# Attention and MLP on one core: a second v product a pair in three passes, two low queries made on GpSimd

## The chip, the core and the metric

The kernel runs on one core of a Trainium2 chip. Its engines are PE (TensorE, matrix products into PSUM; PEld is its weight load), DVE (VectorE), ACT (ScalarE), POOL (GpSimd) and SP (SyncE, which here issues DMAs). The metric is the device time of one execution in microseconds.

## The reference

```python
q_rot, k_rot = (rotate(q), rotate(k))          # rotary embedding, halves of the 64 features
scores = scale * np.matmul(q_rot, k_rot.transpose(0, 1, 3, 2))
scores = scores - np.max(scores, axis=-1, keepdims=True)
attn = np.exp(scores)
attn = attn / (np.sum(attn, axis=-1, keepdims=True) + 1e-09)
out = np.matmul(attn, v)                       # 4 x 8 heads, 576 tokens, 64 features
...
h = x @ w_in                                   # x: 2304 tokens x 512; w_in: 512 x 1024
e = np.exp(h - np.max(h, axis=-1, keepdims=True))
solu = h * (e / (np.sum(e, axis=-1, keepdims=True) + 1e-09))
ln = (solu - mu) / np.sqrt(var + 1e-06) * g_ln
return (ln @ w_out).astype(np.float32)
```

All is fp32.

## The kernel before, in words

**Pairs and steps.** The 32 heads are taken as 16 pairs (n = 0 to 15), head a = 0 on partitions 0 to 63 and a = 1 on 64 to 127. The 576 keys of a head are four blocks of 128 and a tail of 64; the two tails share a block. That makes 9 steps a pair: s = 0 to 3 are the blocks of head 0, s = 4 (BOTH) the tails, s = 5 to 8 the blocks of head 1. In step s PE computes `score(n, s)` (L1014), ACT its exponential (`exp`, L573, the row L593), and PE, one step behind, the product of an earlier exponential with its v block (`weigh`, L1071, the row L1087). The product of step 7's exponential is k = 8 and is made in step 8. The tails' product is `weigh_tails`. Between them PE computes one block of scores of the next pair, row by query (`row_scores(n + 1, s)`, L986, row L1010), from which DVE takes maxima (`row_max`, L771, row L782). All maxima of steady pairs use one PSUM place, so a `row_scores` waits until the maximum before it is taken, on `max_taken`.

**Two numbers for one.** Queries, keys and weights are split into a rounded part and the rest, both of a type that PE takes in one pass: `high` on ACT (L536, row L541) rounds queries and keys of a pair, `second_queries` (L554, row L556) copies the rounded queries to the other head's partitions, `copy_keys` (L559) the rounded keys; `low_keys` (L751, row L757) and `low_queries` (L761, row L767) make the rest on DVE, `w_high` (L604) and `w_low` (L804, row L806) do it for the MLP's weights. The v products are unsplit fp32, two PE records for each half of the columns, but for one block a pair: `halved(n, k)` (L216) is true for k = 3 in pairs 1 to 14. There the exponential goes from one PSUM place to another (L587), ACT rounds it into p_hi (L590), DVE makes p_lo (`low_p`, L792, row L795), GpSimd has made v_hi and v_lo of that block (`halve_v`, L419), and PE runs three passes (`weigh_halves`, L1060, row L1067), after waits for all of these.

**What sets the order.** Nothing schedules at run time. Each engine runs its own list in the order of its loops, and waits on semaphores; whatever stands behind a wait waits with it. GpSimd's loop for pair n (L510) is: wait for `low_q_done[1]` of pair n + 1, multiply pair n + 2 by the rotary table (L394), divide pair n - 2's output (L434), copy the tails (`set_tails`), and `halve_v(n + 1)`. DVE's loop (L904) has, beside the maximum of each step: low_keys(n + 1, 1) in step 0, low_queries(n + 1, 1) in step 1, low_p in step 3, w_low in step 4, the rotary `add(n + 2)` in step 5, the reciprocal (`invert`) in step 6, low_keys(n + 2, 0) in step 7, low_queries(n + 2, 0) in step 8. Pair 1 has its own variants. ACT's loop (L647) has high(n + 2, 0) behind the exponential of step 6 and second_queries(n + 2, 0) behind that of step 7. SP loads the input of pair n + 3 once its buffer's reader counts are reached (`wait_x`, L258).

**After the pairs** come 18 tiles of 128 tokens through the MLP, which the change leaves alone.

Of the kernel before, what the change touches and what calls it, by code (L numbers as in the profile page):

```python
# [52 lines left out]
HALVED = 3  # L53
# [7 lines left out]
def attention_then_mlp(nc: bass.Bass, x_d, v_d, rope_d, w_d, gain_d, out_d):  # L61
# [8 lines left out]
    with ctx:  # L70
# [19 lines left out]
        v_hi = sb("v_hi", [P, P], F32R)  # L90
        v_lo = sb("v_lo", [P, P], F32R)
# [13 lines left out]
        v_hi_done = sem("v_hi_done")  # L105
        v_lo_done = sem("v_lo_done")
# [109 lines left out]
        def halved(n, k):  # L216

            return k == HALVED and 1 <= n < PAIRS - 1

# [37 lines left out]
        def _(sp):  # L257
            def wait_x(m):  # L258
                for a in range(2):
                    sp.wait_ge(hi_done[a], 2 * m - 2)  # L260
                    sp.wait_ge(low_k_done[a], m - 1)
                    sp.wait_ge(low_q_done[a], m - 1)
                if m >= 3:
                    sp.wait_ge(tails_set, 3 * (m - 2))

# [124 lines left out]
        def _(pool):  # L390
# [14 lines left out]

            def set_tails(m):
# [59 lines left out]
            nc.gpsimd.memset(v_hi[:, D:P].bitcast(F32), 1.0).then_inc(v_const, 1)  # L466
            nc.gpsimd.memset(v_lo[:, D:P].bitcast(F32), 0.0).then_inc(v_const, 1)
            pool.wait_ge(v_const, 6)
# [66 lines left out]
        def _(act):  # L535
            def high(m, a):  # L536
# [22 lines left out]
            def copy_keys(m, a):  # L559
# [3 lines left out]
                else:  # L563
                    act.wait_ge(hi_done[a], 2 * m + 1)
# [8 lines left out]
            def exp(n, s):  # L573
# [73 lines left out]
            for n in range(PAIRS):  # L647
                if 2 <= n < PAIRS - 1:
                    high(n + 1, 1)
                for s in range(STEPS):  # L650
                    exp(n, s)
                    if n == 1 and s == 0:
                        high(2, 1)
                    if n == 1 and s == 1:
                        second_queries(2, 1)
                    if n == 0:
                        if s == 2:
                            high(1, 0)
                            second_queries(1, 0)
                        if s == 3:  # L660
                            high(1, 1)
# [55 lines left out]
        def _(dve):  # L717
# [33 lines left out]
            def low_keys(m, a):  # L751
# [3 lines left out]
                else:  # L755
                    dve.wait_ge(hi_done[a], 2 * m + 1)
# [4 lines left out]
            def low_queries(m, a):  # L761
# [3 lines left out]
                if m == 2 and a == 0:  # L765
                    dve.wait_ge(low_q_done[0], 2)
# [25 lines left out]
            def low_p(n):  # L792

                dve.wait_ge(p_hi_done, n)
                nc.vector.tensor_tensor(p_lo[:, :].rearrange("p (b c) -> p b c", b=2), o_ps[1][:, :, 0:HALF],  # L795
# [97 lines left out]
            for s in range(STEPS):  # L893
# [7 lines left out]
                if s == 8:  # L901
                    low_keys(2, 0)
                    low_queries(1, 1)
            for n in range(1, PAIRS - 1):  # L904
                for s in range(STEPS):
# [17 lines left out]
                    if s == 7 and n + 2 < PAIRS:  # L923
# [49 lines left out]
        def _(pe):  # L973
# [12 lines left out]
            def row_scores(m, i):  # L986
                c, k = m % 2, STEPS * m + i
                if i == 0:
                    pe.wait_ge(hi_done[0], 2 * m + 2)
                    pe.wait_ge(low_k_done[0], m + 1)  # L990
                    pe.wait_ge(pool_const, 7)
                if i == BOTH:
                    pe.wait_ge(hi_done[1], 2 * m + 2)
# [66 lines left out]
            def weigh_halves(n):  # L1060

                pe.wait_ge(v_lo_done, n)
                pe.wait_ge(p_hi_done, n)
                pe.wait_ge(p_lo_done, n)
                for v, p in ((v_hi, p_hi), (v_lo, p_hi), (v_hi, p_lo)):
                    for half in range(2):
                        ins = nc.tensor.matmul(o_ps[0][:, half, 0:HALF], v[:, :], p[:, half * HALF:(half + 1) * HALF],  # L1067
# [3 lines left out]
            def weigh(n, k, half):  # L1071
                if halved(n, k):
                    if half == 1:
                        weigh_halves(n)
# [3 lines left out]
                if half == 0:  # L1078
                    if k == 0:
                        pe.wait_ge(v_loaded[c], uses(n) * 32)  # L1080
                        pe.wait_ge(v_const, 6)
# [136 lines left out]
```

## Time and profile before

| | before |
|---|---|
| median of 3 runs | 487.47 us (487.36 to 487.50) |
| the profiled execution's own time | 487.08 us |
| its span | 485.3 us |
| PE busy | 476.8 us (98%) |
| DVE busy | 368.7 us (76%) |
| ACT busy | 264.4 us (54%) |
| POOL busy | 191.9 us (40%) |
| PE's waits named by the profile | 4.8 us in all, none between 85 and 252 us |

The busy time of an engine is read beside the stretch it lies in: ACT's 54% is an average over the pairs, where it is near 80%, and the MLP. The page's chain of work that ended last is PE for 95% of the span. In the timelines each line gives a start, a duration, the engine, the line of the kernel, the operation with its output and inputs, and in brackets the engine's idle time before it with its releaser. PE's durations overlap, as products are pipelined, so the time that one costs is the difference of two starts.

### The profile page before, as it was taken

To read this page: it belongs to the slowest core of one execution; us is meant where nothing else is said; L and a number is where in the kernel's file an instruction comes from. 1 tells how busy PE (TensorE), PEld (TensorE's weight loads), DVE (VectorE), ACT (ScalarE), POOL (GpSimd) and SP (SyncE) were. 2 spreads that over 40 slices of the span, in tenths; PEclk is the share of its full clock that TensorE was granted. 3 is DMA by queue.
4 is the path that set the end of the run, shared out by engine and by line. 5 is a ranking of instruction groups with operands and counts; after the bars stand their busy time and mean duration, and the time that the engine had idled before them with its cause. 6 is when DMAs were issued, how large, how long until landed. Compare 5 with 4: busy or idle time off the path is not lost.

```text
span 485.3 us, 7697 instructions
## 1 busy us (share of the span) xinstructions
PE 476.8 (98%) x2527; PEld 403.1 (83%) x2527; DVE 368.7 (76%) x580; ACT 264.4 (54%) x397; POOL 191.9 (40%) x238
## 2 busy tenths in 40 slices
PE   8899999999999999999999999999999999999997
PEld 7677888988888888888888878888888888888885
DVE  6869787787778777877876356999897899888731
ACT  4667787778788778877787353033224222322221
POOL 6856356536453654565361012343343121122110
PEclk9999999999999999999999999999999999999999
DMA  8503454535454554445424112133333233322332
GB/s 291 188 12 76 138 158 110 178 123 162 117 156 143 144 148 141 155 108 166 149 72 99 39 34 52 32 65 87 81 70 86 47 54 67 80 56 60 62 77 85
DMA packets 101007, 50.58 MB, mean 104 GB/s; under 512 B 90280, under 2 KB 90280, under 8 KB 99048
## 3 DMA queue, kind: packets, MB, share of 16 engines
q1 hardware_dynamic: 100152, 50.00, 38.3%
q8 instruction: 20, 0.33, 0.3%
q10 hardware_dynamic: 816, 0.10, 0.1%
q14 instruction: 19, 0.16, 0.1%
HBM read 33.33 MB, written 4.79 MB: 79 GB/s over the span
## 4 chain that ended last, share of the span: by engine, by line
PE 95%; DVE 2%; ACT 1%; DMA 1%; POOL 1%; issue 0%; SPq 0%; DVEq 0%; POOLq 0%; ACTq 0%
PE ps L1087 22%; PE ps L1101 20%; PE ps L1115 20%; PE ps L1039 18%; PE ps L1010 8%; PE ps L1054 4%; PE ps L1067 2%; DMA X<-x_in 1%; POOL xT L394 1%; DVE nm L782 1%; DVE X L723 1%; DVE X L728 0%; ACT QK L541 0%; ACT p_main L593 0%; ACT QK L556 0%
## 5 line engine op out<-in xcount | busy, mean ns | idle before, releaser
L782 DVE TENSOR_REDUCE nm<-ps 128x1 fp32r<-128x576 f32 x144 | 108.2, 756 | 49.7 <-PE ps L1010 47.4
L1087 PE MATMUL ps<-p_main,V 128*128 128x288 f32 x456 | 129.5, 406 | 0.0
L593 ACT ACTIVATE p_main<-ps 128x576 f32<-128x576 f32 x114 | 74.2, 651 | 39.5 <-PE ps L1039 37.2
L1039 PE MATMUL ps<-QK 128*128 128x288 f32 x320 | 92.9, 371 | 0.8 <-ACT p_main L593 0.5
L394 POOL TENSOR_TENSOR X<-X,rope 128x1152 f32<-128x1152 f32 x26 | 68.7, 2665 | 59.9 <-DVE KB L767 59.7
L1101 PE MATMUL ps<-w_hi,KB 128*128 128x512 f32 x288 | 91.4, 390 | 0.0
L1115 PE MATMUL ps<-w_hi,QK 128*128 128x512 f32 x288 | 90.8, 389 | 0.0
L1087 PEld LDWEIGHTS ps<-p_main,V 128*128 128x128 f32 x456 | 80.3, 190 | 12.2 <-ACT p_main L593 0.2
L1039 PEld LDWEIGHTS ps<-QK 128*128 128x128 f32 x320 | 56.7, 189 | 19.3 <-issue 5.7
L1039 PE MATMUL ps<-KB 128*128 128x288 f32 x320 | 67.7, 293 | 0.0
L614 ACT ACTIVATE X<-ps,neg_max 128x1024 f32<-128x1024 f32 x18 | 20.1, 1119 | 83.3 <-DVE neg_max L827 83.3
L1115 PEld LDWEIGHTS ps<-w_hi,QK 128*128 128x128 f32 x288 | 54.0, 188 | 11.2
L1101 PEld LDWEIGHTS ps<-w_hi,KB 128*128 128x128 f32 x288 | 54.0, 188 | 11.1
L1010 PE MATMUL ps<-QK 128*128 128x288 f32 x260 | 57.2, 304 | 2.3 <-DVE nm L782 1.2
L448 POOL COPY V<-oe 32x256 f32<-32x256 f32 x72 | 29.7, 413 | 74.6 <-DVE QK L833 42.0
L1101 PE MATMUL ps<-w_lo,KB 128*128 128x512 f32 x144 | 56.1, 389 | 0.0
L1115 PE MATMUL ps<-w_lo,QK 128*128 128x512 f32 x144 | 56.0, 389 | 0.0
L1039 PEld LDWEIGHTS ps<-KB 128*128 128x128 f32 x320 | 51.5, 188 | 0.0
L434 POOL TENSOR_TENSOR xT<-xT,inv 128x576 f32<-128x576 f32 x16 | 23.4, 1460 | 60.0 <-DMA inv<-inv_rows 30.5
L1010 PEld LDWEIGHTS ps<-QK 128*128 128x128 f32 x260 | 40.8, 188 | 5.9 <-DVE nm L782 3.3
L438 POOL TENSOR_TENSOR r<-r,expo 128x1 f32<-128x1 f32 x18 | 16.4, 911 | 59.4 <-DVE r L856 59.4
L628 ACT ACTIVATE X<-ps 128x512 f32<-128x512 f32 x18 | 10.7, 596 | 47.7 <-PE ps L1115 42.6
(101 smaller groups left out, 646.8 us busy)
## 6 DMA issues: line engine op xcount, KB each, us to landing
X<-x_in SPq DMA_DIRECT2D x13, 1152.0 KB, 5.2
V<-oe SPq DMA_DIRECT2D x213, 32.0 KB, 1.9
V<-v_in SPq DMA_DIRECT2D x32, 160.0 KB, 2.7
out<-X SPq DMA_DIRECT2D x18, 256.0 KB, 2.3
w_raw<-w_in SPq DMA_DIRECT2D x16, 256.0 KB, 2.9
xT<-x_in SPq DMA_DIRECT2D x2, 1152.0 KB, 10.3
xT<-oe SPq DMA_DIRECT2D x16, 144.0 KB, 2.4
inv<-inv_rows SPq DMA_DIRECT2D x16, 144.0 KB, 2.9
```

Of the source, the lines that this page charges most:

```text
L394: nc.gpsimd.tensor_tensor(x, x, rope[:, :, :], ALU.mult).then_inc(done, 1)
L434: nc.gpsimd.tensor_tensor(xT[:, m, :], xT[:, m, :], inv[:, :], ALU.mult).then_inc(x_done, 1)
L448: nc.gpsimd.tensor_copy(blocks(ln_T[a], group, group), blocks(turned_l[a], group, group))\
L593: nc.scalar.activation(dst[:, :].rearrange("p (b c) -> p b c", b=2), score_ps[:, :, 0:HALF], ACT.Exp, scale=SCALE).then_inc(exp_done, 1)
L614: nc.scalar.activation(e[:, :].rearrange("p (b c) -> p b c", b=2), h_ps[t % 3], ACT.Exp, bias=neg_max[:, a:a + 1], accum_out=total[:, a:a ...
L782: nc.vector.tensor_reduce(nm[g][:, at:at + 1], src[:, :, 0:HALF], AX_XY, ALU.max, negate=True)\
L1010: ins = nc.tensor.matmul(slot[:, half, 0:HALF], queries, keys[:, half * HALF:(half + 1) * HALF], start=(g == 0), stop=(g == len(parts) - 1))
L1039: ins = nc.tensor.matmul(score_ps[:, half, 0:HALF], keys[:, of:of + P], queries[:, to + half * HALF:to + (half + 1) * HALF], start=(g == 0 ...
L1054: ins = nc.tensor.matmul(o_ps[a][:, half, 0:HALF], V[c][own(a), a, 0, :], p_tail[own(a), half * HALF:(half + 1) * HALF], start=(a == 1), s ...
L1087: ins = nc.tensor.matmul(o_ps[a][:, half, 0:HALF], v, p[:, half * HALF:(half + 1) * HALF], start=(k == 0), stop=(k == 9))
L1101: ins = nc.tensor.matmul(h_ps[t % 3][:, half, :], left[a][:, c, :], right[:, col:col + 512], start=(c == 0 and k == 0), stop=(c == KC - 1 ...
L1115: ins = nc.tensor.matmul(y_ps[a], left[a][:, c * P:(c + 1) * P], right[:, col:col + 512], start=(i == 0), stop=(i == DOWNS - 1))
```

## The change

HALVED becomes (3, 8): in pairs 1 to 14 the product k = 8 (the exponential of step 7, head 1) is made in three passes too. Its exponential goes to the other head's output place, o_ps[0]; p_hi and p_lo are shared by both products of a pair, and v_hi, v_lo exist twice. From pair 3 on, second_queries(m, 0) moves from ACT to GpSimd, with a semaphore of its own on which the first `row_scores` of a pair and the loads of x also wait. low_queries(1, 1) and low_queries(2, 0) move from DVE to GpSimd. On DVE, low_keys(n + 2, 0) goes from step 7 to step 6, pair 1's low_keys and low_queries lose their special places, and w_low(0) goes from step 4 of pair 1 to step 6, behind the reciprocal. On GpSimd the division follows the tails and the first halve_v.

```diff
-HALVED = 3
+HALVED = (3, 8)
...
+        def halves(n, a):
+
+            return 2 * (n - 1) + a + 1
+
+        def high(m, a):
+
+            return m + 4 if a == 0 and m >= 3 else 2 * m + 1
+
+        def copied(m, a):
+
+            return m + 4 if a == 0 and m >= 3 else 2 * m + 2
...
+                if m >= 5:
+                    sp.wait_ge(second_done, m - 4)
...
+            def low_queries(m, a):
+
+                c, at = m % 2, COLS[a]
+                nc.gpsimd.tensor_tensor(KB[c][own(a), 1, at:at + S], x_of(m)[own(a), 1, :],
+                                        QK[c][own(a), 0, at:at + S].bitcast(F32), ALU.subtract)\
+                  .then_inc(low_q_done[a], 1)
...
-            def halve_v(m):
+            def halve_v(m, a):
 
                 pool.wait_ge(v_loaded[m % 2], uses(m) * 32)
                 if m >= 2:
-                    pool.wait_ge(pv_done, PVS * (m - 1) + HALVED + 1)
-                    pool.wait_ge(v_lo_done, m - 1)
-                v = V[m % 2][:, 0, 1 + HALVED, 0:D]
-                nc.gpsimd.tensor_copy(v_hi[:, 0:D], v).then_inc(v_hi_done, 1)
-                pool.wait_ge(v_hi_done, m)
-                nc.gpsimd.tensor_tensor(v_lo[:, 0:D], v, v_hi[:, 0:D].bitcast(F32), ALU.subtract).then_inc(v_lo_done, 1)
-                pool.wait_ge(v_lo_done, m)
+                    pool.wait_ge(pv_done, PVS * (m - 1) + HALVED[a] + 1)
+                    pool.wait_ge(v_lo_done[a], m - 1)
+                v = V[m % 2][:, a, (HALVED[1] - 5 if a else HALVED[0] + 1), own(a)]
+                nc.gpsimd.tensor_copy(v_hi[a][:, own(a)], v).then_inc(v_hi_done[a], 1)
+                pool.wait_ge(v_hi_done[a], m)
+                nc.gpsimd.tensor_tensor(v_lo[a][:, own(a)], v, v_hi[a][:, own(a)].bitcast(F32), ALU.subtract)\
+                  .then_inc(v_lo_done[a], 1)
+                pool.wait_ge(v_lo_done[a], m)
+
+            def second_queries(m):
+
+                pool.wait_ge(score_ready, STEPS * (m - 2) + BOTH + 1)
+                nc.gpsimd.tensor_copy(QK[m % 2][other(0), 0, 0:S], x_of(m)[own(0), 1, :]).then_inc(second_done, 1)
+                pool.wait_ge(second_done, m - 2)
...
             pool.wait_ge(rot_done, 3)
-            nc.gpsimd.tensor_tensor(KB[1][own(0), 1, 0:S], x_of(1)[own(0), 1, :], QK[1][own(0), 0, 0:S].bitcast(F32),
-                                    ALU.subtract).then_inc(low_q_done[0], 1)
+            low_queries(1, 0)
+            pool.wait_ge(hi_done[1], 3)
+            pool.wait_ge(low_q_done[1], 1)
+            low_queries(1, 1)
+            pool.wait_ge(hi_done[0], 5)
+            pool.wait_ge(low_q_done[0], 2)
+            low_queries(2, 0)
             pool.wait_ge(low_q_done[0], 3)
             set_tails(2)
-            halve_v(1)
+            halve_v(1, 0)
+            halve_v(1, 1)
             for n in range(1, PAIRS):
                 if n + 2 < PAIRS:
                     pool.wait_ge(low_q_done[1], n + 2)
@@ -515,14 +551,16 @@
                     else:
                         pool.wait_ge(x_loaded[n % 2], uses(n + 2) * 16 - (16 if n % 2 else 32))
                     rotate(n + 2)
+                if n + 2 < PAIRS:
+                    pool.wait_ge(rot_done, n + 3)
+                    second_queries(n + 2)
+                    set_tails(n + 2)
+                if halved(n + 1, HALVED[0]):
+                    halve_v(n + 1, 0)
                 if n >= 2:
-                    if n + 2 < PAIRS:
-                        pool.wait_ge(rot_done, n + 3)
                     divide(n - 2)
-                if n + 2 < PAIRS:
-                    set_tails(n + 2)
-                if halved(n + 1, HALVED):
-                    halve_v(n + 1)
+                if halved(n + 1, HALVED[1]):
+                    halve_v(n + 1, 1)
...
-                if s < BOTH and halved(n, s):
-                    act.wait_ge(o_taken, 2 * n)
-                    nc.scalar.activation(o_ps[1][:, :, 0:HALF], score_ps[:, :, 0:HALF], ACT.Exp, scale=SCALE)\
+                if s != BOTH and halved(n, s + s // BOTH):
+                    a = s // BOTH
+                    act.wait_ge(o_taken, 2 * n + a)
+                    nc.scalar.activation(o_ps[1 - a][:, :, 0:HALF], score_ps[:, :, 0:HALF], ACT.Exp, scale=SCALE)\
                       .then_inc(exp_done, 1)
                     act.wait_ge(exp_done, STEPS * n + s + 1)
-                    nc.scalar.activation(p_hi[:, :].rearrange("p (b c) -> p b c", b=2), o_ps[1][:, :, 0:HALF], ACT.Copy)\
-                      .then_inc(p_hi_done, 1)
+                    nc.scalar.activation(p_hi[:, :].rearrange("p (b c) -> p b c", b=2), o_ps[1 - a][:, :, 0:HALF],
+                                         ACT.Copy).then_inc(p_hi_done, 1)
...
                     if s == (7 if n == 0 else 6) and n + 2 < PAIRS:
-                        high(n + 2, 0)
-                    if s == (8 if n == 0 else 7) and n + 2 < PAIRS:
-                        second_queries(n + 2, 0)
+                        set_high(n + 2, 0)
+                    if n == 0 and s == 8:
+                        second_queries(2, 0)
...
                     low_keys(2, 0)
-                    low_queries(1, 1)
             for n in range(1, PAIRS - 1):
                 for s in range(STEPS):
                     for place in range(3):
                         for i in maxima(n, s)[place]:
                             row_max(n + 1, i)
-                    if n == 1 and s == 0:
-                        low_queries(2, 0)
-                    if s == (1 if n == 1 else 0):
+                    if s == 0:
                         low_keys(n + 1, 1)
-                    if s == (2 if n == 1 else 1):
+                    if s == 1:
                         low_queries(n + 1, 1)
-                    if s == 4:
+                    if s == 4 and n >= 2:
                         w_low(n - 1)
-                    if s == 3 and halved(n, HALVED):
-                        low_p(n)
+                    if s == 3 and halved(n, HALVED[0]):
+                        low_p(n, 0)
+                    if s == 7 and halved(n, HALVED[1]):
+                        low_p(n, 1)
                     if s == 5 and n + 2 < PAIRS:
                         add(n + 2)
                     if s == 6:
                         invert(n - 1)
-                    if s == 7 and n + 2 < PAIRS:
+                        if n == 1:
+                            w_low(0)
+                    if s == 6 and n + 2 < PAIRS:
                         low_keys(n + 2, 0)
...
-                    pe.wait_ge(hi_done[0], 2 * m + 2)
+                    pe.wait_ge(hi_done[0], copied(m, 0))
+                    if m >= 3:
+                        pe.wait_ge(second_done, m - 2)
...
+            def weigh_halves(n, a):
+
+                pe.wait_ge(v_lo_done[a], n)
+                pe.wait_ge(p_hi_done, halves(n, a))
+                pe.wait_ge(p_lo_done, halves(n, a))
+                for v, p in ((v_hi[a], p_hi), (v_lo[a], p_hi), (v_hi[a], p_lo)):
                     for half in range(2):
-                        ins = nc.tensor.matmul(o_ps[0][:, half, 0:HALF], v[:, :], p[:, half * HALF:(half + 1) * HALF],
+                        ins = nc.tensor.matmul(o_ps[a][:, half, 0:HALF], v[:, :], p[:, half * HALF:(half + 1) * HALF],
                                                start=False, stop=False)
                 ins.then_inc(pv_done, 1)
```

DVE's list in pair 2, from the maximum of step 5 on; nm is written by a maximum, QK by low_keys, KB by low_queries, p_lo by low_p, sc by the reciprocal. Before:

```order
L782 TENSOR_REDUCE nm<-ps 128x1
L749 TENSOR_TENSOR X<-X 128x2x576
L782 TENSOR_REDUCE nm<-ps 128x1
L802 RECIPROCAL sc<-sc 128x9
L782 TENSOR_REDUCE nm<-ps 128x1
L757 TENSOR_TENSOR QK<-X,QK 64x576
L782 TENSOR_REDUCE nm<-ps 128x1
L790 STREAM_TRANSPOSE nm_row<-nm 128x32
L767 TENSOR_TENSOR KB<-X,QK 64x576
```

and of the change:

```order
L788 TENSOR_TENSOR X<-X 128x2x576
L821 TENSOR_REDUCE nm<-ps 128x1
L841 RECIPROCAL sc<-sc 128x9
L796 TENSOR_TENSOR QK<-X,QK 64x576
L821 TENSOR_REDUCE nm<-ps 128x1
L834 TENSOR_TENSOR p_lo<-ps,p_hi 128x576
L821 TENSOR_REDUCE nm<-ps 128x1
L829 STREAM_TRANSPOSE nm_row<-nm 128x32
L806 TENSOR_TENSOR KB<-X,QK 64x576
```

low_keys has passed the maximum of step 7, and low_p stands between that maximum and the one of step 8.

ACT's list in the same place, from the take-over of head 0's output (oe) on. Before:

```order
L601 ACTIVATE oe<-ps 128x576
L593 ACTIVATE p_main<-ps 128x576
L541 ACTIVATE QK<-X 64x2x576
L593 ACTIVATE p_main<-ps 128x576
L556 ACTIVATE QK<-X 64x576
L593 ACTIVATE p_main<-ps 128x576
```

and of the change:

```order
L640 ACTIVATE oe<-ps 128x576
L632 ACTIVATE p_main<-ps 128x576
L579 ACTIVATE QK<-X 64x2x576
L626 ACTIVATE ps<-ps 128x2x288
L629 ACTIVATE p_hi<-ps 128x576
L632 ACTIVATE p_main<-ps 128x576
```

The copy into p_hi stands where second_queries stood.

GpSimd's list at the start, from the second rotary product of pair 2 to that of pair 3; the numbers in the names are buffers (1 is pair 1's and pair 3's). Before:

```order
L394 TENSOR_TENSOR xT<-xT,rope 128x1152
L505 TENSOR_TENSOR KB1<-X1,QK1 64x576
L412 CAST tail_k<-xT 128x576
L414 CAST tail_q<-xT 64x64
L416 CAST tail_q<-xT 64x64
L426 CAST v_hi<-V1 128x64
L428 TENSOR_TENSOR v_lo<-V1,v_hi 128x64
```

and of the change:

```order
L409 TENSOR_TENSOR xT<-xT,rope 128x1152
L424 TENSOR_TENSOR KB1<-X1,QK1 64x576 x2
L424 TENSOR_TENSOR KB0<-xT,QK0 64x576
L434 CAST tail_k<-xT 128x576
L436 CAST tail_q<-xT 64x64
L438 CAST tail_q<-xT 64x64
L448 CAST v_hi_a<-V1 128x64
L450 TENSOR_TENSOR v_lo_a<-V1,v_hi_a 128x64
L448 CAST v_hi_b<-V1 128x64
L450 TENSOR_TENSOR v_lo_b<-V1,v_hi_b 128x64
```

Two subtractions and the second v block's pair have come in ahead of pair 3's rotary product.

## Rows read from the trace of the kernel before

**Rows 1.** One stretch with all engines' busy time; columns: engine, busy us (instructions), clock, DMA.

```profile
85.00:252.00 167.00, 167.00 (x1004) 145.67 (x1002) 130.12 (x191) 132.71 (x202) 87.98 (x82) 1.00 0.48 143
```

**Rows 2.** The timeline of PE, one pair; start us, us, engine, line, operation.

```profile
112.24 0.42 PE L1067 MATMUL ps<-p_hi,v_hi 128*128 128x288 f32 x2
...
113.03 0.43 PE L1039 MATMUL ps<-QK 128*128 128x288 f32 x2
113.30 0.42 PE L1039 MATMUL ps<-KB 128*128 128x288 f32 x2
...
118.52 0.64 PE L1039 MATMUL ps<-QK 128*128 128x288 f32 x2
119.00 0.42 PE L1039 MATMUL ps<-KB 128*128 128x288 f32 x2
119.26 0.43 PE L1010 MATMUL ps<-QK 128*128 128x288 f32 x2
119.53 1.13 PE L1087 MATMUL ps<-p_main,V 128*128 128x288 f32 x4
120.28 0.64 PE L1039 MATMUL ps<-QK 128*128 128x288 f32 x2
120.76 0.42 PE L1039 MATMUL ps<-KB 128*128 128x288 f32 x2
```

**Rows 3.** The timeline of ACT, the same pair.

```profile
109.86 0.64 ACT L587 ACTIVATE ps<-ps 128x576 f32<-128x576 f32 x1 [0.41 <-PE ps L1039]
110.53 0.65 ACT L590 ACTIVATE p_hi<-ps 128x576 fp32r<-128x576 f32 x1
...
116.47 1.15 ACT L541 ACTIVATE QK<-X 64x1152 fp32r<-64x1152 f32 x1
117.69 0.65 ACT L593 ACTIVATE p_main<-ps 128x576 f32<-128x576 f32 x1
118.36 0.69 ACT L556 ACTIVATE QK<-X 64x576 fp32r<-64x576 f32 x1
```

**Rows 4.** The timeline of DVE, the same pair.

```profile
111.21 0.76 DVE L795 TENSOR_TENSOR p_lo<-ps,p_hi 128x576 fp32r<-128x576 f32 x1 [0.32 <-ACT p_hi L590]
...
113.46 0.75 DVE L806 SCALAR_TENSOR_TENSOR w_lo<-w_raw,gain,w_hi 128x512 fp32r<-128x512 f32 x1
...
116.87 0.20 DVE L802 RECIPROCAL sc<-sc 128x9 f32<-128x9 f32 x1
117.96 0.76 DVE L782 TENSOR_REDUCE nm<-ps 128x1 fp32r<-128x576 f32 x1 [0.89 <-PE ps L1010]
118.75 0.75 DVE L757 TENSOR_TENSOR QK<-X,QK 64x576 fp32r<-64x576 f32 x1
```

**Rows 5.** The timeline of DVE, one other pair, the slowest of this row.

```profile
168.73 0.98 DVE L757 TENSOR_TENSOR QK<-X,QK 64x576 fp32r<-64x576 f32 x1
```

**Rows 6.** The timeline of POOL there.

```profile
168.44 0.66 POOL L412 CAST tail_k<-X 128x576 fp32r<-128x576 f32 x1
```

**Rows 7.** The timeline of PE at the start of pair 1 and in it.

```profile
36.87 0.50 PE L1010 MATMUL ps<-QK 128*128 128x288 f32 x2
...
48.83 0.54 PE L1010 MATMUL ps<-QK 128*128 128x288 f32 x2 [0.89 <-DVE nm L782]
49.20 1.13 PE L1087 MATMUL ps<-p_main,V 128*128 128x288 f32 x4
```

**Rows 8.** The timeline of DVE there.

```profile
36.02 0.75 DVE L757 TENSOR_TENSOR QK<-xT,QK 64x576 fp32r<-64x576 f32 x1
...
45.51 2.60 DVE L806 SCALAR_TENSOR_TENSOR w_lo<-w_raw,gain,w_hi 128x512 fp32r<-128x512 f32 x1
```

**Rows 9.** The timeline of POOL at the start.

```profile
32.34 1.41 POOL L505 TENSOR_TENSOR KB<-X,QK 64x576 fp32r<-64x576 f32 x1 [2.56 <-DVE xT L743]
...
44.92 2.64 POOL L394 TENSOR_TENSOR xT<-xT,rope 128x1152 f32<-128x1152 f32 x1
```

**Rows 10.** The page's costliest groups: GpSimd's products with the rotary table, and its waits.

```profile
L394 POOL TENSOR_TENSOR X<-X,rope 128x1152 f32<-128x1152 f32 x26 | 68.7, 2665 | 59.9 <-DVE KB L767 59.7
```

More of the change, by code:

```diff
@@ L89, in attention_then_mlp @@
         p_lo = sb("p_lo", [P, S], F32R)
-        v_hi = sb("v_hi", [P, P], F32R)
-        v_lo = sb("v_lo", [P, P], F32R)
+        v_hi = [sb(f"v_hi_{h}", [P, P], F32R) for h in "ab"]
+        v_lo = [sb(f"v_lo_{h}", [P, P], F32R) for h in "ab"]
         oe = [sb(f"oe{c}", [P, 2, S]) for c in range(2)]
@@ L104, in attention_then_mlp @@
         p_lo_done = sem("p_lo_done")
-        v_hi_done = sem("v_hi_done")
-        v_lo_done = sem("v_lo_done")
+        v_hi_done = [sem(f"v_hi_{h}_done") for h in "ab"]
+        v_lo_done = [sem(f"v_lo_{h}_done") for h in "ab"]
+        second_done = sem("second_done")
         x_loaded = [sem(f"x_loaded{c}") for c in range(2)]
@@ L216, in halved @@
         def halved(n, k):
-            return k == HALVED and 1 <= n < PAIRS - 1
+            return k in HALVED and 1 <= n < PAIRS - 1
+        def halves(n, a):
[4 more added lines that the diff above has]
+            return m + 4 if a == 0 and m >= 3 else 2 * m + 2
         def last_pair(t):
@@ L259, in wait_x @@
                 for a in range(2):
-                    sp.wait_ge(hi_done[a], 2 * m - 2)
+                    sp.wait_ge(hi_done[a], copied(m - 2, a))
                     sp.wait_ge(low_k_done[a], m - 1)
@@ L465, in _ @@
                 nc.gpsimd.memset(V[c][:, 1, :, 0:D], 1.0).then_inc(v_const, 1)
-            nc.gpsimd.memset(v_hi[:, D:P].bitcast(F32), 1.0).then_inc(v_const, 1)
-            nc.gpsimd.memset(v_lo[:, D:P].bitcast(F32), 0.0).then_inc(v_const, 1)
-            pool.wait_ge(v_const, 6)
+            for a in range(2):
+                nc.gpsimd.memset(v_hi[a][:, other(a)].bitcast(F32), 1.0).then_inc(v_const, 1)
+                nc.gpsimd.memset(v_lo[a][:, other(a)].bitcast(F32), 0.0).then_inc(v_const, 1)
+            pool.wait_ge(v_const, 8)
             nc.gpsimd.memset(expo[:, :], -0.5).then_inc(const_done, 1)
@@ L535, in _, with set_high @@
         def _(act):
-            def high(m, a):
+            def set_high(m, a):
                 c, at = m % 2, COLS[a]
@@ L563, in copy_keys @@
                 else:
-                    act.wait_ge(hi_done[a], 2 * m + 1)
+                    act.wait_ge(hi_done[a], high(m, a))
                 nc.scalar.activation(KB[c][own(a), 0, at:at + S], QK[c][own(a), 1, at:at + S].bitcast(F32), ACT.Copy)\
@@ L648, in _ @@
                 if 2 <= n < PAIRS - 1:
-                    high(n + 1, 1)
+                    set_high(n + 1, 1)
                 for s in range(STEPS):
@@ L652, in _ @@
                     if n == 1 and s == 0:
-                        high(2, 1)
+                        set_high(2, 1)
                     if n == 1 and s == 1:
@@ L657, in _ @@
                         if s == 2:
-                            high(1, 0)
+                            set_high(1, 0)
                             second_queries(1, 0)
                         if s == 3:
-                            high(1, 1)
+                            set_high(1, 1)
                         if s == 4:
@@ L755, in low_keys @@
                 else:
-                    dve.wait_ge(hi_done[a], 2 * m + 1)
+                    dve.wait_ge(hi_done[a], high(m, a))
                 nc.vector.tensor_tensor(QK[c][other(a), 1, at:at + S], x_of(m)[own(a), 3, :],
@@ L764, in low_queries @@
                     dve.wait_ge(hi_done[a], 2)
-                if m == 2 and a == 0:
-                    dve.wait_ge(low_q_done[0], 2)
+                if m == 2 + (1 - a):
+                    dve.wait_ge(low_q_done[a], m)
                 nc.vector.tensor_tensor(KB[c][own(a), 1, at:at + S], x_of(m)[own(a), 1, :],
@@ L790, in row_max, with low_p @@
                     nc.vector.transpose(nm_row[g][:, :], nm[g][:, :].bitcast(F32)).then_inc(turned[g], 1)
-            def low_p(n):
-                dve.wait_ge(p_hi_done, n)
-                nc.vector.tensor_tensor(p_lo[:, :].rearrange("p (b c) -> p b c", b=2), o_ps[1][:, :, 0:HALF],
+            def low_p(n, a):
+                dve.wait_ge(p_hi_done, halves(n, a))
+                nc.vector.tensor_tensor(p_lo[:, :].rearrange("p (b c) -> p b c", b=2), o_ps[1 - a][:, :, 0:HALF],
                                         p_hi[:, :].bitcast(F32).rearrange("p (b c) -> p b c", b=2), ALU.subtract)\
@@ L992, in row_scores @@
                 if i == BOTH:
-                    pe.wait_ge(hi_done[1], 2 * m + 2)
+                    pe.wait_ge(hi_done[1], copied(m, 1))
                     pe.wait_ge(low_k_done[1], m + 1)
@@ L1058, in weigh_tails @@
                             ins.then_inc(pv_done, 1)
[L1060 to L1065, printed above, removed]
+            def weigh_halves(n, a):
[3 more added lines that the diff above has]
+                for v, p in ((v_hi[a], p_hi), (v_lo[a], p_hi), (v_hi[a], p_lo)):
                     for half in range(2):
-                        ins = nc.tensor.matmul(o_ps[0][:, half, 0:HALF], v[:, :], p[:, half * HALF:(half + 1) * HALF],
+                        ins = nc.tensor.matmul(o_ps[a][:, half, 0:HALF], v[:, :], p[:, half * HALF:(half + 1) * HALF],
                                                start=False, stop=False)
@@ L1073, in weigh @@
                     if half == 1:
-                        weigh_halves(n)
+                        weigh_halves(n, k // 5)
                     return
@@ L1080, in weigh @@
                         pe.wait_ge(v_loaded[c], uses(n) * 32)
-                        pe.wait_ge(v_const, 6)
+                        pe.wait_ge(v_const, 8)
                         pe.wait_ge(max_taken, STEPS)
```

## The prediction, made before the result was known

> **What bounds the kernel now.** I read the table of busy time by stretches first. From 85 to 252 us PE is busy 167.00 of 167.00 us at the full granted clock, while DVE has 130, ACT 133 and POOL 88 [rows 1]. So in the attention part every microsecond of a pair is PE's; the other engines count only where PE would have to stand for them. The timeline of PE gives the price of each piece, the difference between one start and the next. The timelines of ACT and DVE in the same pair give the chain that makes the three-pass product's operands. Last come the start of pair 1, where PE does stand [rows 7], and what GpSimd waits for [rows 10].
>
> **The saving of a second product in halves.** An ordinary v product takes 119.53 to 120.28 = 0.75, and the score row behind it 0.48 (120.28 to 120.76) [rows 2]. The product in three passes takes 112.24 to 113.03 = 0.79, and the row behind it only 0.27 (113.03 to 113.30). So 1.23 becomes 1.06: 0.17 saved in each of 14 pairs (1 to 14), 2.4 us if nothing waits. Between 0 and 2.4 the rows leave no other reading, as both forms stand in the same pair.
>
> **What it needs, and when.** The product for block 8 is due at 119.53, right behind score(n,8) (118.52) and the key-row product of the next pair (119.26) [rows 2]. Its exponential is that of step 7, which starts at 117.69 [rows 3], as soon as score(n,7) is there. In the existing case the exponential starts at 109.86, its rounded copy at 110.53, the difference on DVE at 111.21, ending 111.97 [rows 3, 4]: 2.11 us from start to end. Step 4 gives that case cover, because score(n,4) has two sets of passes and the halves come at 112.24. Step 8 has one set: 117.69 + 2.11 = 119.80, and PE is ready at 119.53. So the cover is too short by 0.27 even with a free DVE.
>
> DVE is not free. The order of before has maximum(7), then low_keys(n+2,0), at 117.96 and 118.75 [rows 4]. The change puts low_keys in step 6, ahead of maximum(7). It must wait for ACT's rounding of that pair, 116.47 + 1.15 = 117.62 [rows 3], long after the reciprocal ends at 117.07 [rows 4]. So low_keys runs 117.65 to 118.40, maximum(7) 118.43 to 119.19 instead of 117.96 to 118.72, low_p 119.22 to 119.98. (ACT's copy ends 118.36 + 0.65 = 119.01, earlier.) Both maxima and low_p are queued behind the waiting low_keys, and PE waits for both: the key-row product at 119.26 needs maximum(7), taken by 119.25, just in time; the halves need low_p, 0.06 after its end (0.03 to 0.1: ACT to DVE is 0.03 in [rows 3, 4], DVE's end at 36.77 to PE's start at 36.87 is 0.1 in [rows 7, 8]): 120.04. After a wait PE's first pair of passes takes 0.37, not 0.26 (48.83 to 49.20 [rows 7]; 0.26 from 119.00 to 119.26 without one [rows 2]). So three passes 0.90, the next score row's first 0.27: 121.21 against 120.76. **Each of pairs 2 to 13 loses 0.45 net, 12 x 0.45 = 5.4 us.** Bounds for one pair: +0.17 (no wait of DVE and no slower restart: 119.86 + 0.79 + 0.27 = 120.92) and +0.68 (low_keys at 0.98, its slowest row [rows 5], instead of 0.75). I take the middle, since 0.75 is the usual duration. Pair 14 has no low_keys: 119.86 + 0.90 + 0.27 = 121.03, +0.27.
>
> **ACT, at nothing.** Its second_queries (0.69 at 118.36 [rows 3]) goes from exactly the place where the copy of 0.65 comes. exp(8) at 119.46 is not touched.
>
> **GpSimd in the steady pairs, at nothing.** It gets second_queries (64x576, one input), a second rounding and difference of a v block, and the division comes after the first rounding. It stands idle 59.7 us in 12 waits for low_queries ahead of its rotary products [rows 10], about 5 a pair. The three new operations are not in the trace; each is no larger than its subtraction of 64x576 with two inputs, 1.41 [rows 9], so together at most 4.2, which fits (and at least nothing); I take them as covered. second_queries(n+2) is needed only by the first key-row product of the next pair. Were this cover gone, the next add would come late and with it ACT's rounding. The x loads' added wait in SP is for the same rounding a pair earlier. The two extra small fills at the start lie in GpSimd's idle time.
>
> **The start.** The weights' difference w_low(0) stands at 45.51 and takes 2.60 [rows 8], beside GpSimd's product that runs to 47.56 [rows 9]; in a steady pair it takes 0.75, at 113.46 [rows 4]. PE therefore idles 0.89 at 48.83, and restarts 0.10 slower [rows 7]. Moving it behind the reciprocal takes this away: -0.99. But two subtractions of 1.41 each [rows 9] now follow the one at 32.34 on GpSimd: 33.8 to 35.2 and 35.3 to 36.7. DVE's low_keys(2,0), at 36.02 [rows 8], falls into the second. By the w_low row, which ended 0.55 after GpSimd's, it ends at 37.25 instead of 36.77; PE's product at 36.87 [rows 7] is waiting for it: +0.5 (bounds 0 and 0.7). Start together -0.5.
>
> In words of the Trainium skill, GPSIMD Engine Reference, section 1 (Specifications): the engine shares its SBUF interfaces with VectorE and contends with VectorE instructions that have two SBUF inputs. The 2.60 us row agrees. By that rule the queries made on GpSimd are not a free relief for DVE but hold up low_keys(2,0); without it the start would be worth -0.99 and not -0.5.
>
> Pair 1 in its step 6 has w_low(0) of 0.75 between the reciprocal and low_keys. It fills the 0.55 in which DVE would wait for ACT (117.07 to 117.62) and runs 0.2 over: 0.45 + 0.2 = +0.65.
>
> **Sum.** 5.4 + 0.27 + 0.65 - 0.5 = +5.8 on the profiled execution's own 487.08 (span 485.3 and 1.78 around it): 492.9. The median of the runs is 0.39 above it, which would make 493.3; I say 493.0. In the second part of the program PE goes on without waits, so the shift arrives whole.
>
> **Rivals.**
> - *DVE in time*: low_keys gets done before it matters, and only the short cover of step 8 is left. For it: pair 14 is so. Against: ACT's rounding ends at 117.62 by its row. 14 x 0.27 = 3.8, less 0.5: 490.4. Chance 0.17.
> - *Contention in the loop*: low_keys now meets GpSimd's casts each time and takes 0.98. For it: the slow row [rows 5] begins beside such a cast [rows 6]. Against: 0.75 in most pairs beside the same work. 13 pairs at 0.68, pair 14 0.27, pair 1 0.2 more, less 0.5: +8.8, 495.9. Chance 0.13.
> - *Faster*: the halves of block 8 find their operands ready. It decides in favour once low_p ends by 119.47, 0.5 before what I work out; then 14 x 0.17 and 0.5 are saved: 484.2. For it: the first halves never wait in the trace. Against: they have a step of twice the scores ahead of them. Chance 0.09.
> - *Nothing comes of it*, gains and waits cancel: 487. Chance 0.03.
> - *Larger*: GpSimd becomes late with second_queries or with the v halves, and the first key-row product waits as well, 1 us a pair: above 498. Chance 0.04.
> - My forecast, 0.54; its own range is 491.6 to 494.4 (0.1 a pair either way).
>
> A change of under 0.2% (1 us) can't be told from none here. Faster has 0.09, within 0.2% 0.04, slower 0.87. The range 489.5 to 497 takes in the first two rivals and leaves out some 0.16.
>
> **What would show it.** PE waiting some 0.5 us ahead of the halves of block 8 with low_p as the releaser, in 14 pairs; a DVE order of low_keys, maximum(7), low_p without idle time; a pair's time on PE up by 0.45 us; no wait of 0.89 in pair 1 but a later first key-row product of pair 2. PE without those waits and pairs 0.17 us shorter would prove me wrong.

## The result, and the profile after

The changed kernel takes 492.24 us (median of 6 runs, 492.05 to 492.57), the kernel before 487.48 (6 runs beside it): ratio 1.0097, 95% interval 1.0086 to 1.0107. It is slower by 4.8 us. The profiled execution has a span of 490.2 us against 485.3.

From the page of the changed kernel, the busy time and the chain that ended last:

```profile
PE 477.9 (97%) x2555; PEld 403.7 (82%) x2555; DVE 376.8 (77%) x592; ACT 263.9 (54%) x398; POOL 218.9 (45%) x283
...
PE 84%; DVE 8%; ACT 4%; issue 2%; DMA 1%; SPq 0%; ACTq 0%; DVEq 0%
```

PE's busy time has hardly moved (477.9 against 476.8, and overlapping durations blur it), but the chain, 95% PE before, now runs for 8% through DVE and for 4% through ACT. PE's waits in the changed kernel (engine, line, waited for; us in total, times, longest):

```profile
PE ps L1109 <- DVE p_lo L834: 3.2, 14, 0.3
PE ps L1052 <- ACT QK L589: 1.5, 1, 1.5
...
PE ps L1052 <- DVE nm L821: 0.6, 2, 0.3
...
PE ps L1052 <- issue: 0.5, 1, 0.5
```

There is one new wait in 14 pairs: the three-pass product (L1109) for p_lo. Where before none stood between 85 and 252 us [rows 1], each pair has one, of 0.22 us in the steady pairs. The timeline of PE, steps 4 and 8 of a steady pair of the changed kernel:

```profile
113.47 0.42 PE L1109 MATMUL ps<-p_hi,v_hi_a 128*128 128x288 f32 x2
113.73 0.43 PE L1109 MATMUL ps<-p_hi,v_lo_a 128*128 128x288 f32 x2
114.00 0.42 PE L1109 MATMUL ps<-p_lo,v_hi_a 128*128 128x288 f32 x2
114.27 0.43 PE L1081 MATMUL ps<-QK 128*128 128x288 f32 x2
114.54 0.42 PE L1081 MATMUL ps<-KB 128*128 128x288 f32 x2
...
119.75 0.64 PE L1081 MATMUL ps<-QK 128*128 128x288 f32 x2
120.23 0.42 PE L1081 MATMUL ps<-KB 128*128 128x288 f32 x2
120.49 0.53 PE L1052 MATMUL ps<-QK 128*128 128x288 f32 x2
121.25 0.50 PE L1109 MATMUL ps<-p_hi,v_hi_b 128*128 128x288 f32 x2 [0.22 <-DVE p_lo L834]
121.58 0.42 PE L1109 MATMUL ps<-p_hi,v_lo_b 128*128 128x288 f32 x2
121.84 0.43 PE L1109 MATMUL ps<-p_lo,v_hi_b 128*128 128x288 f32 x2
122.11 0.42 PE L1081 MATMUL ps<-QK 128*128 128x288 f32 x2
122.37 0.42 PE L1081 MATMUL ps<-KB 128*128 128x288 f32 x2
```

The product of block 3 at 113.47 is as [rows 2] has it: 0.80 to the next score row, which takes 0.27. The one of block 8 ought to follow the key-row product at 120.49 by 0.27 and comes 0.76 behind it, so 0.49 late, of which the record names 0.22 as idle. From score(n,8) to the second part of the next score row, 119.75 to 122.37, is 2.62 us, where [rows 2] has 118.52 to 120.76 = 2.24. ACT and DVE in the same pair:

```profile
117.71 1.15 ACT L579 ACTIVATE QK<-X 64x1152 fp32r<-64x1152 f32 x1
118.92 0.64 ACT L626 ACTIVATE ps<-ps 128x576 f32<-128x576 f32 x1
119.59 0.65 ACT L629 ACTIVATE p_hi<-ps 128x576 fp32r<-128x576 f32 x1
```

```profile
117.43 0.76 DVE L821 TENSOR_REDUCE nm<-ps 128x1 fp32r<-128x576 f32 x1
118.11 0.21 DVE L841 RECIPROCAL sc<-sc 128x9 f32<-128x9 f32 x1
118.89 0.75 DVE L796 TENSOR_TENSOR QK<-X,QK 64x576 fp32r<-64x576 f32 x1 [0.58 <-ACT QK L579]
119.68 0.76 DVE L821 TENSOR_REDUCE nm<-ps 128x1 fp32r<-128x576 f32 x1
120.35 0.75 DVE L834 TENSOR_TENSOR p_lo<-ps,p_hi 128x576 fp32r<-128x576 f32 x1
121.06 0.76 DVE L821 TENSOR_REDUCE nm<-ps 128x1 fp32r<-128x576 f32 x1
```

On DVE low_keys (L796) waits 0.58 us for ACT's rounding, and behind it stand the maximum and low_p without a gap; low_p ends at 121.10 and PE starts at 121.25. This answers to [rows 3, 4], where DVE was idle 0.89 us ahead of the maximum. Counted from one product of block 3 to the next, a pair takes 17.03 us (17.00 to 17.04 in 12 intervals) instead of 16.66.

### The profile page after: what moved, and what is told of

Its sections match the earlier page's. It is cut to its first block, busy times and chain, and to the rows that moved or that the text cites. A ratio compares the mean times of both kernels' runs of the same rounds, so it can differ in the third digit from the quotient of the medians.

```text
span 490.2 us, 7879 instructions
## 1 busy us (share of the span) xinstructions
PE 477.9 (97%) x2555; PEld 403.7 (82%) x2555; DVE 376.8 (77%) x592; ACT 263.9 (54%) x398; POOL 218.9 (45%) x283
## 4 chain that ended last, share of the span: by engine, by line
PE 84%; DVE 8%; ACT 4%; issue 2%; DMA 1%; SPq 0%; ACTq 0%; DVEq 0%
PE ps L1143 20%; PE ps L1157 20%; PE ps L1081 15%; PE ps L1129 14%; PE ps L1052 6%; PE ps L1109 5%; PE ps L1096 4%; ACT QK L579 3%; DVE nm L821 3%; DVE QK L796 2%; DVE p_lo L834 2%; DMA X<-x_in 1%; DVE X L762 1%; ACT p_main L632 0%; DVE X L767 0%
## 5 line engine op out<-in xcount | busy, mean ns | idle before, releaser
L1129 PE MATMUL ps<-p_main,V 128*128 128x288 f32 x400 | 113.6, 406 | 0.0
L1081 PE MATMUL ps<-QK 128*128 128x288 f32 x320 | 89.8, 362 | 0.8 <-ACT p_main L632 0.5
L632 ACT ACTIVATE p_main<-ps 128x576 f32<-128x576 f32 x100 | 65.0, 650 | 43.5 <-PE ps L1081 42.2
L1129 PEld LDWEIGHTS ps<-p_main,V 128*128 128x128 f32 x400 | 70.4, 190 | 10.7 <-ACT p_main L632 0.2
L1081 PEld LDWEIGHTS ps<-QK 128*128 128x128 f32 x320 | 55.9, 189 | 17.8 <-issue 5.7
L1052 PE MATMUL ps<-QK 128*128 128x288 f32 x260 | 58.2, 308 | 2.9 <-ACT QK L589 1.5
L1052 PEld LDWEIGHTS ps<-QK 128*128 128x128 f32 x260 | 40.6, 188 | 7.1 <-DVE nm L821 2.5
L866 DVE TENSOR_REDUCE neg_max<-ps 128x1 f32<-128x1024 f32 x18 | 21.6, 1199 | 19.2 <-PE ps L1143 19.2
```

What stands on the lines that cost most here:

```text
L632: nc.scalar.activation(dst[:, :].rearrange("p (b c) -> p b c", b=2), score_ps[:, :, 0:HALF], ACT.Exp, scale=SCALE).then_inc(exp_done, 1)
L866: nc.vector.tensor_reduce(neg_max[:, a:a + 1], h_ps[t % 3], AX_XY, ALU.max, negate=True)\
L1052: ins = nc.tensor.matmul(slot[:, half, 0:HALF], queries, keys[:, half * HALF:(half + 1) * HALF], start=(g == 0), stop=(g == len(parts) - 1))
L1081: ins = nc.tensor.matmul(score_ps[:, half, 0:HALF], keys[:, of:of + P], queries[:, to + half * HALF:to + (half + 1) * HALF], start=(g == 0 ...
L1129: ins = nc.tensor.matmul(o_ps[a][:, half, 0:HALF], v, p[:, half * HALF:(half + 1) * HALF], start=(k == 0), stop=(k == 9))
```

## The experiments

All are timed beside the kernel before (medians 487.31 to 487.37); "a pair" is the distance on PE from block 3's product to the next pair's, over the 12 steady intervals.

**The wait by itself.** PE's wait for p_lo is moved behind the passes that don't read it:

```diff
-                pe.wait_ge(p_lo_done, halves(n, a))
                 for v, p in ((v_hi[a], p_hi), (v_lo[a], p_hi), (v_hi[a], p_lo)):
+                    if p is p_lo:
+                        pe.wait_ge(p_lo_done, halves(n, a))
                     for half in range(2):
```

> The changed kernel, with PE's wait for p_lo moved behind the first two of the three passes, in both products of a pair. Theory A (the loss is PE's wait for low_p, 0.22 us of idle plus a slower restart in each of 14 pairs): the first two passes need only p_hi, which is there 0.5 us before they are due; the third is due 0.53 after the first, and low_p ends about then, so nothing waits, each pair goes from +0.38 to -0.17 against the kernel before, 14 x 0.55 = 7.7 less than 492.2: 484.5. Rival B (the loss comes with the work moved onto GpSimd and the order of DVE, and the wait only shows it): a wait turns up elsewhere and it stays at 491 to 492.5. Rival C (three passes are no cheaper than the fp32 product in this place): the wait goes, the saving does not come, 487.

Measured: 485.74 us, ratio to before 0.9969 (0.9957 to 0.9981); a pair 16.57. The wait for p_lo is gone and none came elsewhere. So the one new wait was worth 6.5 us, more than the whole loss, and rival B falls; so does rival C, with a time 1.3 below its 487. It is 1.2 short of the 7.7 expected. PE in that kernel:

```profile
118.67 0.42 PE L1081 MATMUL ps<-KB 128*128 128x288 f32 x2
118.93 0.53 PE L1052 MATMUL ps<-QK 128*128 128x288 f32 x2
119.29 0.42 PE L1110 MATMUL ps<-p_hi,v_hi_b 128*128 128x288 f32 x2
119.56 0.43 PE L1110 MATMUL ps<-p_hi,v_lo_b 128*128 128x288 f32 x2
119.83 0.42 PE L1110 MATMUL ps<-p_lo,v_hi_b 128*128 128x288 f32 x2
120.09 0.43 PE L1081 MATMUL ps<-QK 128*128 128x288 f32 x2
```

The three passes run at 0.27 each. But the key-row product ahead of them takes 0.36 (118.93 to 119.29) where before it took 0.27: I read it as a wait for the maximum of step 7 without idle time in the record; the kernel with one product, below, tests that. It is the 0.09 by which the pair is 16.57 and not 16.49. No run took it out of the kernel with two products.

**What the passes cost with everything ready.** DVE's low_p(n, 1) is left out and the third pass of block 8 reads block 3's p_lo, so this part of the output isn't computed:

```diff
-                    if s == 7 and halved(n, HALVED[1]):
-                        low_p(n, 1)
...
-                pe.wait_ge(p_lo_done, halves(n, a))
+                pe.wait_ge(p_lo_done, n)
```

> The changed kernel without low_p for block 8: the third pass takes the p_lo of block 3 of the same pair, so that its part of the output is left wrong, and waits for nothing new. It shows what the passes cost when their operands are ready. Theory A: 14 x 0.55 less than the changed kernel, 484.5, the same as with the late wait within 0.3. If the late wait is slower than this by more, its third pass still waits. Rival C: 487.

Measured: 485.72 us (0.9967, 0.9955 to 0.9980); a pair 16.57 on average. That is the time of the late wait, so there the third pass waits for nothing (low_p ends at 119.54, the third pass starts at 119.83).

**The moves without the product.** Block 8 is fp32 again. What else the change moved stays, but for GpSimd's rounding of the second v block, which from pair 2 on goes with the product:

```diff
-            return k in HALVED and 1 <= n < PAIRS - 1
+            return k == HALVED[0] and 1 <= n < PAIRS - 1
...
-            return 2 * (n - 1) + a + 1
+            return n
```

> The changed kernel with the three passes for block 3 only, so block 8 is an fp32 product as before; the moves on ACT, DVE and GpSimd, the division of the v blocks and the start all stay as changed. Theory A: 487.0, the kernel before less 0.5 for the start, since the maximum of step 7 is late by 0.5 but still in time for PE. Rival B (the moved work costs the time): 490 to 492.

Measured: 487.89 us (1.0013, 1.0004 to 1.0022); a pair 16.74. Both had missed: the moves cost 0.08 a pair, which theory A had at nothing and rival B far higher. The second product with its operands ready is worth 16.74 - 16.57 = 0.17 a pair, as [rows 2] gave. What the 0.08 is, was tried with low_keys back in its old place of this kernel:

```diff
-                    if s == 6 and n + 2 < PAIRS:
+                    if s == 7 and n + 2 < PAIRS:
                         low_keys(n + 2, 0)
```

> The changed kernel with one product in halves (487.9, 0.08 us a pair above the kernel before), and low_keys(n + 2, 0) back in step 7 of DVE's list. If the 0.08 is PE's key-row product of step 8 waiting for the maximum of step 7, which low_keys holds up, a pair is back at 16.66 us and the time 12 x 0.08 = 1.0 lower: 486.9. Rival (the work moved onto GpSimd costs it): 487.9.

Measured: 486.29 us (0.9981, 0.9972 to 0.9989); a pair 16.66. The 0.08 was low_keys ahead of the maximum, 1.0 us in 12 pairs, and the queries copied on GpSimd cost nothing in the loop. Another 0.5 came in pair 1, whose interval went from 17.15 to 16.64: there w_low(0) and low_keys both stood ahead of the maximum.

**low_keys behind low_p**, the same edit as above, made to the changed kernel with its two products:

> The changed kernel, with DVE's low_keys(n + 2, 0) back in step 7, here behind low_p of block 8. Theory A says that low_keys ahead of the maximum of step 7 makes low_p 0.18 later: PE waits that much less, 13 x 0.18 = 2.3, so 489.9; but low_keys now stands ahead of the maximum of step 8, and the next pair's first key-row product can wait for that, 0.15 a pair, which leaves 491.8. So 489.9 to 491.8, with the wait ahead of the halves down from 0.22 to about 0.05. Rival: low_p is not held up by low_keys at all but by ACT's copy; then the wait stays 0.22 and the time 492.2 or above.

Measured: 499.07 us (1.0243, 1.0229 to 1.0257); a pair 17.63. Theory A missed by over 7 us. The rival had the wait right, which stayed, but has no reason for a time so far above 492. The waits on PE:

```profile
PE ps L1052 <- DVE nm L821: 5.7, 13, 0.5
PE ps L1109 <- DVE p_lo L834: 3.6, 14, 0.3
```

The wait for p_lo did not go, since the chain got only 0.07 shorter (2.11 from the exponential's start to the end of low_p, against 2.18 in the changed kernel) and low_p now waits for ACT's copy; the halves come 0.69 behind the key-row product ahead of them instead of 0.76. And a second wait came: the next pair's key-row product for the maximum of step 8. DVE and GpSimd there:

```profile
121.85 0.76 DVE L834 TENSOR_TENSOR p_lo<-ps,p_hi 128x576 fp32r<-128x576 f32 x1 [0.32 <-ACT p_hi L629]
122.64 1.17 DVE L796 TENSOR_TENSOR QK<-X,QK 64x576 fp32r<-64x576 f32 x1
123.84 0.76 DVE L821 TENSOR_REDUCE nm<-ps 128x1 fp32r<-128x576 f32 x1
```

```profile
121.78 1.43 POOL L463 TENSOR_TENSOR xT<-xT,inv 128x576 f32<-128x576 f32 x1
```

low_keys takes 1.17 us instead of 0.75, and ends 0.6 after GpSimd's division (two inputs, to 123.21) does. Whether the one makes the other was tried by moving the division away from it:

```diff
                     second_queries(n + 2)
+                if n >= 2:
+                    divide(n - 2)
+                if n + 2 < PAIRS:
                     set_tails(n + 2)
                 if halved(n + 1, HALVED[0]):
                     halve_v(n + 1, 0)
-                if n >= 2:
-                    divide(n - 2)
```

> The kernel with low_keys(n + 2, 0) behind low_p of block 8 (499.1), and GpSimd's division ahead of its tail copies, as in the kernel before. If low_keys took 1.17 instead of 0.75 there because GpSimd's two-input division runs beside it, it is back near 0.75 and each pair gains 0.4: 17.63 to 17.2 us, 494. If it is the place in DVE's list alone, it stays at 499.

Measured: 494.05 us (1.0137, 1.0122 to 1.0153); a pair 17.21. low_keys is back at 0.75 and 0.42 a pair is gained; its rows:

```profile
121.43 0.75 DVE L797 TENSOR_TENSOR QK<-X,QK 64x576 fp32r<-64x576 f32 x1
122.21 0.76 DVE L822 TENSOR_REDUCE nm<-ps 128x1 fp32r<-128x576 f32 x1
```

```profile
118.54 1.42 POOL L463 TENSOR_TENSOR xT<-xT,inv 128x576 f32<-128x576 f32 x1
```

So of the 6.8 us above the changed kernel, 5.0 were the meeting with the division and 1.8 the place in DVE's list.

**The start.** w_low(0) alone moved in the kernel before:

```diff
-                    if s == 4:
+                    if s == 4 and n >= 2:
                         w_low(n - 1)
...
                         invert(n - 1)
+                        if n == 1:
+                            w_low(0)
```

> The kernel before with one edit: w_low(0) behind the reciprocal of pair 1's step 6. Theory A: the 2.60 us row goes and with it PE's 0.89 of idle time and 0.10 of slower restart: 486.5 against 487.4. Rival: another DVE instruction meets GpSimd's product instead, and it stays at 487.4.

Measured: 486.54 us (0.9982, 0.9974 to 0.9991), 0.8 below before where 0.9 was expected; pair 1 went from 17.97 to 16.94. With the two low queries made on GpSimd as well (the change's own lines on GpSimd and DVE):

> The kernel before with the whole start of the change: w_low(0) moved, low_queries(1, 1) and low_queries(2, 0) on GpSimd; one product in halves, nothing moved in the loop. Theory A: low_keys(2, 0) on DVE is stretched from 0.75 to 1.3 by GpSimd's second subtraction and PE's first key-row product of pair 2 comes 0.5 later, so 0.3 to 0.5 slower than with the weights alone: 486.9. Rival: DVE's relief is worth more than the stretch, at or below 486.5.

Measured: 486.30 us (0.9979, 0.9970 to 0.9987). Not told apart from the one before by the intervals, 0.2 lower by the medians, so the rival had the number and the 0.4 more of theory A is not in the time. In the trace it is: low_keys(2, 0) takes 1.30, and counted from DVE's first maximum the first halves of pair 1 come 0.40 later (12.05 to 44.78, against 12.46 to 44.79). Against it stand pair 1, shorter by 0.28 (16.94 to 16.66), since DVE's add of pair 3 no longer waits 0.82 for GpSimd's rotary products, and a first maximum that lay 0.41 earlier in this profile, which I can't put down to the edit.

With both products and the late wait, the two low queries back on DVE (the same lines undone):

> The changed kernel with the late wait for p_lo, and the two low queries of the start back on DVE; w_low(0) stays behind the reciprocal. Theory A: 0.3 to 0.5 below 485.7, so 485.3. Rival: DVE is short of time in pair 1 with its second low_p, and it comes out at 485.7 or above.

Measured: 486.85 us (0.9987, 0.9978 to 0.9996), 1.1 above the late wait alone: the rival had the number, but not the cause. DVE isn't short of time, its add of pair 3 waits for GpSimd:

```profile
48.91 1.36 DVE L782 TENSOR_TENSOR xT<-xT 128x1152 f32<-128x1152 f32 x1 [1.57 <-POOL xT L409]
```

```profile
50.99 0.53 PE L1049 MATMUL ps<-QK 128*128 128x288 f32 x2 [0.79 <-DVE nm L815]
...
53.65 0.53 PE L1049 MATMUL ps<-QK 128*128 128x288 f32 x2 [0.63 <-DVE nm L815]
```

```profile
39.72 0.67 POOL L434 CAST tail_k<-xT 128x576 fp32r<-128x576 f32 x1 [5.44 <-DVE KB L800]
...
43.53 5.28 POOL L409 TENSOR_TENSOR xT<-xT,rope 128x1152 f32<-128x1152 f32 x2
```

GpSimd's tail copies of pair 2 wait 5.44 us for low_queries(2, 0), which DVE makes again, and two v blocks stand behind them now; so the rotary products of pair 3 begin at 43.53 instead of 42.03 (in the late wait alone). DVE's add waits for them 1.57 us and PE twice for maxima queued behind it. Two steps from here, each on top of the late wait. First, GpSimd's low_queries(2, 0) held back until DVE's low_keys(2, 0) is done:

```diff
             pool.wait_ge(low_q_done[0], 2)
+            pool.wait_ge(low_k_done[0], 3)
             low_queries(2, 0)
```

> The changed kernel with the late wait for p_lo, and one more wait on GpSimd: its low_queries(2, 0) begins only when DVE's low_keys(2, 0) is done. If low_keys(2, 0) takes 1.3 instead of 0.75 us because GpSimd's two-input subtraction runs beside it, it is back at 0.75 and the time is 485.2, 0.5 below the late wait alone. If the stretch has another cause it stays 1.3 and 485.7.

Measured: 485.63 us (0.9964, 0.9951 to 0.9976), 0.1 below the late wait and not told apart from it. The stretch is gone:

```profile
36.15 0.75 DVE L797 TENSOR_TENSOR QK<-xT,QK 64x576 fp32r<-64x576 f32 x1
```

and PE's first key-row product of pair 2 comes at 37.00 instead of 37.96 (0.37 of it from an earlier beginning, before DVE's first maximum); but the rotary products end later, add waits 0.77 for them, and PE 0.62 in step 8 of pair 1. The expected 0.5 was given back there. Second, GpSimd's second v block of pair 1 behind those products, since block 8 is not needed before step 8:

```diff
             halve_v(1, 0)
-            halve_v(1, 1)
...
                     rotate(n + 2)
+                if n == 1:
+                    halve_v(1, 1)
```

> The kernel with the late wait and the later low query, and GpSimd's rounding of the second v block of pair 1 moved behind its rotary products of pair 3. With the later query DVE's add of pair 3 waited 0.77 us for those products and PE then 0.62 in step 8 of pair 1. If GpSimd's list ahead of the rotary products is what is late, they come 0.6 earlier, DVE's add waits 0.2 or less, and the time is 0.5 below 485.6: 485.1. Rival: w_low(0) ahead of low_keys(3, 0) makes the same wait anyway, 485.6.

Measured: 484.91 us, ratio 0.9951 (0.9938 to 0.9963), the fastest by the medians: 2.5 us below the kernel before and 7.3 below the change, though its interval still meets the last one's. Pair 1 went from 17.61 to 16.97. DVE's add starts at 46.84, 0.74 earlier, and waits for nothing.

## Why the prediction was right

**The forecast** was 493.0, slower by 5.5 to 5.8, for one reason: the operands of block 8's product can't be ready in time in a step with one set of scores. That is what the trace shows and what the late wait showed by taking only this wait away. Step by step:

- *The saving*, 0.17 a pair: measured as 16.74 - 16.57 = 0.17.
- *The chain and the loss*, +0.45 in each of 12 pairs: measured 17.03 - 16.66 = 0.37, so 4.5 us instead of 5.4. The mechanism held and three sizes were off. low_keys holds up low_p by 0.07 (2.18 against 2.11) and not by 0.18, since low_p starts 0.67 after the maximum's start where I had added 0.79. PE starts 0.15 after low_p's end, not 0.06. And the restart after the wait takes 0.33, not 0.37. The first alone would be 0.11 less, the second 0.09 more, the third 0.04 less.
- *"Just in time"* for the key-row product of step 8 was wrong by 0.09: it is late. In the changed kernel that lies inside the wait for p_lo and costs nothing; with that wait gone it is what is late next.
- *Pair 14*, +0.27: the stretch from its block 3 to the end of the span grew by 0.31 (223.12 to 223.43).
- *Pair 1*, +0.65 less the 0.99 of w_low(0), so -0.34: measured 17.44 - 17.97 = -0.53.
- *The start*, +0.5 by low_keys(2, 0): it took 1.29, where 1.23 was worked out from the w_low row, and the first halves come 0.66 later. 0.30 of this was already there when DVE began its maxima (12.25 against 11.95 us), a place that lies between 11.95 and 12.46 in these profiles, also in kernels with an unchanged beginning; the rest, 0.36, is what is left for the stretch less DVE's relief. That the whole comes near the +0.5 is in part chance.
- *GpSimd and ACT at nothing*: right. The last kernel with one product has 16.66 a pair with the queries copied on GpSimd. What it lacks, the second v block and ACT's second copy, shows no wait in the late wait kernel: there no wait of PE names GpSimd in the loop, and ACT stands 0.45 us for PE ahead of its next exponential.

The terms add up: 0.66 - 0.53 + 4.46 + 0.31 = 4.9, the difference of the spans, where the forecast's own made 5.8; nearly all of the gap lies in the steady pairs.

**Which part of the chain.** The 0.45 was 0.27 for a step too short even with a free DVE, and 0.18 for low_keys. Pair 14, which has no low_keys, shows the first part by itself. In the changed kernel and, below it, in the kernel before:

```profile
273.05 0.64 PE L1081 MATMUL ps<-QK 128*128 128x288 f32 x2
...
273.79 0.43 PE L1052 MATMUL ps<-QK 128*128 128x288 f32 x2
274.48 0.50 PE L1109 MATMUL ps<-p_hi,v_hi_b 128*128 128x288 f32 x2 [0.25 <-DVE p_lo L834]
...
275.61 0.43 PE L1081 MATMUL ps<-KB 128*128 128x288 f32 x2
```

```profile
268.46 0.64 PE L1039 MATMUL ps<-QK 128*128 128x288 f32 x2
...
270.70 0.42 PE L1039 MATMUL ps<-KB 128*128 128x288 f32 x2
```

That is 2.56 against 2.24 us, a loss of 0.32, where the same stretch of a pair with low_keys loses 0.38. So the short step makes nearly all of the loss, and low_keys under 1 us in 12 pairs. The rival with DVE in time, put at 490.4, would with these sizes stand only some 0.8 us below what was measured. That low_keys is not in time is shown by its wait of 0.58 us for ACT in each of the 12 pairs; the time alone would hardly have told the two apart.

The rival with contention would have had 495.9. low_keys took 0.75 to 0.76 in the steady pairs, so it fell, but by a margin that the forecast had not worked out: in the pair shown GpSimd's cast of 128x576 ends at 118.83 and low_keys starts at 118.89, and the cast of 64x64 beside it is itself the one that takes longer, 0.85 instead of 0.23. The mechanism is real in these kernels: low_keys took 1.17 beside the division and 1.29 beside the subtraction, and 1.10 (at 51.70, in the late wait with the old low queries) beside a cast of 128x576, which has one input. The Trainium skill (GPSIMD Engine Reference, section 1, Specifications) says that GpSimd shares its SBUF interfaces with VectorE and contends with VectorE instructions that have two SBUF inputs; low_keys is one, and these three rows agree.

## What to carry to other kernels

Where a product in several passes waits for several operands, put each wait ahead of the first pass that reads it: here the same instructions in the same order went from 492.2 to 485.7 us by it. Before work is put into a step, compare the length of the chain that makes its operands with what PE has to do in that step, not with the engines' shares of busy time; DVE at 77% and ACT at 54% said nothing of it. And give a large operation on GpSimd a place where VectorE has none with two SBUF inputs, if work that PE waits for is queued behind it: a stretch of 0.42 us cost 5.0 us in the 12 pairs with low_keys back, while undoing the one of 0.55 at the start gave 0.1, since another wait took its place.

## What of the hardware was not expected

A wait that ends in time by the record can still cost: with the late wait PE's key-row product of step 8 shows no idle time, but the next product follows after 0.36 instead of 0.27 us; in the kernel with one product the same 0.08 a pair went when the maximum it needs came earlier. And VectorE's stretch beside GpSimd's work: 0.75 us became 1.17 beside a division of 1.43, 1.29 to 1.31 beside a subtraction of 1.40 in the profiles with that order, and 1.10 beside a one-input cast of 1.14. In the first two cases it was 0.75 again when the two were kept apart; the third was not tried.
